# TensorE filler matmuls in the token routing, and MLP row groups written out in place of a loop

## What is computed

```python
scores = scale * q @ k.T            # 8 heads of 64; heads 0-3: last 32 keys, heads 4-7: every 4th of last 128
x = softmax(scores, mask) @ v       # -> (2304, 512)
expert_idx = argmax(logits); gate_w = softmax(logits)[expert_idx]     # logits: normalised x times 8 normalised rows / tau
y = gate_w * (relu(x @ w1[e]) @ w2[e])      # one of 8 experts per token, hidden width 1024
h = y @ w_in; out = (h * cos(h)) @ w_out    # hidden width 2048
```

## Time and profile before

| What | Value |
|---|---|
| Median of three runs | 880.99 us |
| The profiled execution, its own time | 879.44 us |
| Its span, first to last instruction | 877.5 us |
| Time outside the span (879.44 - 877.5) | 1.9 us |
| TensorE (PE) busy | 823.3 us, 94% |
| TensorE weight loads (PEld) busy | 745.4 us, 85% |
| VectorE (DVE) busy | 607.6 us, 69% |
| ScalarE (ACT) busy | 481.4 us, 55% |
| GpSimd (POOL) busy | 75.6 us, 9% |
| Mean granted TensorE clock | 0.978 |
| Share of TensorE in the chain that ended last | 78% |

### The profile page before, as it was taken

The page is one execution under the profiler, slowest core; times in us unless marked ns, Lnnn a source line. Parts: engine busy times, 40 slices in busy tenths (PEclk is TensorE's granted clock), DMA queues, the critical chain, the costliest instruction groups (busy, mean ns, idle before and its releaser), DMA issues.

```text
span 877.5 us, 15798 instructions
## 1 busy us (share of the span) xinstructions
PE 823.3 (94%) x4902; PEld 745.4 (85%) x4902; DVE 607.6 (69%) x1169; ACT 481.4 (55%) x919; POOL 75.6 (9%) x134
## 2 busy tenths in 40 slices
PE   5999999749999999999989999999999999999993
PEld 3787876439999999999988999988999988999992
DVE  6888886575555566455567777778777788777762
ACT  3557765315545545444456666676656676656651
POOL 4022112141001000000000000001000002000002
PEclk9999999959999999999999999999999999999998
DMA  6498986234444443444242122123212214121001
GB/s 138 93 221 181 193 198 184 70 109 156 129 165 163 144 129 119 139 144 144 73 145 73 49 73 71 51 63 130 72 49 71 72 48 145 48 72 59 14 0 72
DMA packets 114911, 93.67 MB, mean 107 GB/s; under 512 B 65816, under 2 KB 94488, under 8 KB 114848
## 3 DMA queue, kind: packets, MB, share of 16 engines
q1 hardware_dynamic: 109920, 78.81, 31.1%
q0 software_dynamic: 4928, 14.16, 4.9%
HBM read 83.51 MB, written 9.44 MB: 106 GB/s over the span
## 4 chain that ended last, share of the span: by engine, by line
PE 78%; DVE 7%; DMA 5%; issue 4%; ACT 3%; POOL 1%; DVEq 0%; ACTq 0%; POOLq 0%; SPq 0%
PE bank L687 23%; PE bank L689 23%; PE bank L688 23%; DMA xtok<-x_rows 3%; PE bank L585 2%; PE bank L564 2%; PE bank L638 2%; PE bank L729 1%; PE bank L573 1%; DMA x_rows<-osb 1%; PE bank L654 1%; PE bank L548 1%; ACT yh L1010 1%; DMA dn_raw<-in_moe_w_out_dram 1%; DVE row_max L1156 1%
## 5 line engine op out<-in xcount | busy, mean ns | idle before, releaser
L687 PE MATMUL bank<-yh,up_l 128*128 128x384 f32 x384 | 129.7, 338 | 2.4 <-DVE yl L1409 2.4
L689 PE MATMUL bank<-yh,up_h 128*128 128x384 f32 x384 | 130.1, 339 | 0.0
L688 PE MATMUL bank<-yl,up_h 128*128 128x384 f32 x384 | 129.4, 337 | 0.0
L687 PE MATMUL bank<-dn_h,hid 128*128 128x512 f32 x288 | 113.0, 392 | 4.5 <-DVE hid L1431 4.2
L689 PE MATMUL bank<-dn_h,hid 128*128 128x512 f32 x288 | 113.9, 395 | 0.0
L688 PE MATMUL bank<-dn_l,hid 128*128 128x512 f32 x288 | 113.7, 395 | 0.0
L1219 DVE TENSOR_TENSOR dn_l<-dn_raw,dn_h 128x512 fp32r<-128x512 f32 (+1 forms) x80 | 71.9, 900 | 53.3 <-ACT dn_h L905 53.3
L1025 ACT ACTIVATE work<-bank 128x384 f32<-128x384 f32 x96 | 47.2, 491 | 81.4 <-PE bank L689 78.4
L687 PE MATMUL bank<-xh,up_l 128*128 128x352 f32 x256 | 85.2, 333 | 1.7 <-DVE xl L1351 1.4
L1037 ACT ACTIVATE work<-work 128x384 f32<-128x384 f32 x96 | 50.4, 525 | 66.0 <-DVE work L1426 66.0
L1421 DVE TENSOR_SCALAR work<-work 128x384 f32<-128x384 f32 x96 | 34.5, 360 | 75.3 <-ACT work L1025 75.3
(11 more groups left out here) (194 smaller groups left out, 1659.1 us busy)
## 6 DMA issues: line engine op xcount, KB each, us to landing
up_raw<-in_moe_w_dram SPq DMA_DIRECT2D x32, 512.0 KB, 3.5
dn_raw<-in_moe_w_dram SPq DMA_DIRECT2D x32, 512.0 KB, 3.4
up_raw<-in_moe_w_in_dram SPq DMA_DIRECT2D x24, 512.0 KB, 3.2
dn_raw<-in_moe_w_out_dram SPq DMA_DIRECT2D x24, 512.0 KB, 3.4
qn<-in_q_dram SPq DMA_DIRECT2D x32, 144.0 KB, 2.8
kn<-in_k_dram SPq DMA_DIRECT2D x32, 144.0 KB, 3.3
xtok<-x_rows SPq DMA_DIRECT2D x4, 1152.0 KB, 7.5
x_rows<-osb POOLq DMA_DIRECT2D x8, 288.0 KB, 3.9
```

Of the source, the lines that this page charges most:

```text
L687: mm(o, w[1], x[0], start=first, stop=False, skip_group_check=True)
L688: mm(o, w[0], x[1], start=False, stop=False, skip_group_check=True)
L689: return mm(o, w[0], x[0], start=False, stop=last, skip_group_check=True)
```

## The change

Two edits. A helper `fill(n)` on TensorE issues n matmuls of the 128x128 float32 identity by itself into the first 128 columns of bank 4, which nobody reads. It is called at seven places of the routing, always between one step of TensorE and the next wait. And the three loops over m of the MLP become Python loops, so that the body stands in the program three times and each `If` on m is decided when the program is written.

```diff
         def before_this(eng, i, work):
 
+            if isinstance(i, int):
+                if i > 0:
+                    work()
+                return
             with eng.If(i > 0):
                 work()
...
             last.then_inc(logits_done, 1)
 
+            def fill(n):
+
+                for _ in range(n):
+                    mm(bank[4][:, 0:P], ident[:], ident[:], start=True, stop=True, skip_group_check=True)
+
+            fill(14)
             pe.wait_ge(onehot_ready, 1)
...
             mm(bank[5][:, RT * E:2 * RT * E], ones[:], oh, start=True, stop=True, skip_group_check=True).then_inc(counts_done, 1)
 
+            fill(48)
             for t in range(RT):
                 if t % LANE_TILES == 0:
                     pe.wait_ge(lanes_ready, t // LANE_TILES + 1)
...
             last.then_inc(row_ids_done, 1)
+            fill(28)
             pe.wait_ge(to_gate_ready, 1)
...
             last.then_inc(row_gates_done, 1)
+            fill(6)
...
             for tile in range(3):
                 transpose_rows(tile, tile)
+                fill((16, 2, 6)[tile])
             expert_block(0, 0)
...
-            with pe.Fori(0, NM) as m:
+            for m in range(NM):
                 for i in range(2 * FT2):
                     if i >= 2:
                         mlp_up(m, i)
                         mlp_dn(m, i - 2)
                     else:
-                        with pe.If(m > 0):
+                        if m > 0:
                             mlp_up(m, i)
                             mlp_dn(m, i - 2)
...
-            with act.Fori(0, NM) as m:
+            for m in range(NM):
...
-            with dve.Fori(0, NM) as m:
+            for m in range(NM):
```

More of the change, by code:

```diff
@@ L1008, in group_hi @@
             def group_hi(m, half):
-                m = m if isinstance(m, int) else within(m, NM - 1, "under m < NM - 1")
                 A(yh[half][:], X[:, :, bass.ds(m * MR + half * HR, HR)], ACT.Copy).then_inc(ml["in_hi"], 1)
@@ L1075, in _ @@
                     if i in (2 * FT2 - 3, 2 * FT2 - 1):
-                        with act.If(m < NM - 1):
+                        if m < NM - 1:
                             group_hi(m + 1, (i - 2 * FT2 + 3) // 2)
@@ L1088, in _ @@
                     if i == 0:
-                        with act.If(m < 1):
+                        if m < 1:
                             last_block_out()
@@ L1465, in _ @@
                     if i in (2 * FT2 - 3, 2 * FT2 - 1):
-                        with dve.If(m < NM - 1):
+                        if m < NM - 1:
                             group_lo(m + 1, (i - 2 * FT2 + 3) // 2)
@@ L1478, in _ @@
                     if i == 0:
-                        with dve.If(m < 1):
+                        if m < 1:
                             last_block_out()
```

## The result

| | Before | After |
|---|---|---|
| Median | 879.46 us (877.73 to 881.51, 8 runs) | 887.25 us (883.59 to 890.51, 8 runs) |
| The profiled execution, its span | 879.44, 877.5 us | 885.73, 883.9 us |
| Mean granted clock | 0.978 | 0.992 |

The ratio is 1.0085, 95% interval 1.0061 to 1.0108: slower. The direction was right and 887.25 lies in the range. The 2.25 us to the forecast of 885.0 hide larger misses of both signs: as a difference, 4.95 us were forecast, and the medians give 7.8.

A forecast was written before the change was run, and what follows sets the result against it. TensorE bounds the MLP; VectorE's chain and the gathering DMA bound the routing. Routing +5.55, clock +1.6 and loops -2.2 give +4.95 on 879.44, so 884.4, raised to 885.0 us partway toward the median 880.99; range 879.5 to 889.5.

The forecast's parts named there:

- The price of a fill: TensorE in the routing: each fill is two records of 0.109 us, 0.218 us in all.
- Both rivals of other prices: Routing fills: one record of 0.109 us or cheaper, about 877.5 us, chance 0.13; or 0.285 us, about 892, chance 0.09.
- The fills one by one, up to the gates: Routing on TensorE: fills overshoot their waits, making the counts 0.5 us late, the row numbers 2.5 and `gates` 5.4.
- `gates` stands at 192.3: Routing, after fill(28) and 24 matmuls: `gates` is ready at 192.3 instead of 186.85, late by 5.4 us.
- `fill(16)`, 3.49 us, at the full clock: Routing, between the transposes of tiles 0 and 1: the fill runs from 193.85 to 197.35.
- A new idle, and the clock: Before hidden tile 2: TensorE idles some 3.3 us, then a low-clock stretch of 3.4 us costs +1.6 us.
- the case without a fall: Rival for the new idle: no second fall of the clock, +3.35 us, about 883.3 us, chance 0.26.
- The loops, -2.2 us: MLP written out: two back edges give 2 x 1.0 us, register waits at the first group perhaps 0.2.
- Its rival, that nothing comes: MLP loops: 0 instead of -2.2 us, about 887 us, within the first case's range; no chance of its own.
- The whole low stretch is worth about 0.5 us: Routing: 27.3 us at the low clock cost only about 0.5 us on the path.
- The sum: Whole kernel: 5.55 + 1.6 - 2.2 = +4.95 us, from 879.44 to 884.4, stated as 885.0 us.

The follow-up runs named there:

- half_fills: The changed kernel with every count of fills halved (7, 24, 14, 3 and 8, 1, 3), MLP groups written out: 879.51 us, 1.0008 of before.
- repeat_after: The changed kernel once more, unchanged, for a second trace: 887.47 us, 1.0091 of the kernel before.
- fills_only: The changed kernel with its fills kept but the MLP's hardware loops restored: 892.33 us, 1.0145 of the kernel before.
- no_fill_behind_gates: The changed kernel without the fill(6) between row_gates_done and the first transposes: 888.59 us, 1.0111 of the kernel before.
- loops_only: The changed kernel without any fills, MLP groups written out: 876.34 us, 0.9970 of the kernel before.
- early_half: The changed kernel with only the first two fill calls, halved to fill(7) and fill(24), groups written out: 874.29 us, 0.9951 of the kernel before.
- wide_fills: The changed kernel with float32 fills of 512 columns, counts 2, 6, 4, 1 and 2, 0, 1: 876.67 us, 0.9975 of the kernel before.
- short_fills: The changed kernel with bf16 fills of 96x96 by 96 columns, counts 36, 128, 72, 16 and 40, 6, 16: 877.81 us, 0.9981 of before.
- transpose_fills: The changed kernel with full counts, each fill a float32 transpose of the identity, one record: 878.13 us, 0.9985 of the kernel before.

## Why the prediction was right, and where not

- **The price of a fill: right.** The trace holds 5142 - 4902 = 240 more records, two for each. 28 of them take 3.39 us, so (3.39 - 0.27) / 27 = 0.116 a record, and 96 give (10.91 - 0.27) / 95 = 0.112: 0.224 to 0.23 us a fill against my 0.218. Both rivals of other prices fall. By the 134 cycles a matmul of the Trainium skill, "TensorE: Matmul & The Clock Gate", section "Back-to-back issue gap", 0.056 us, 48 fills would take 2.7 us (an estimate), and 10.91 were measured. The same section calls that figure too low for a stream of weight loads and matmuls and gives about 81 ns there, which would be 3.9 us for the 48 (an estimate too).
- **The fills one by one, up to the gates: right.** Less the 1.0 us of the late start, the counts stood at 174.0 (forecast 173.8), VectorE took the row numbers at 185.8 (185.4), and the second 24 began at 191.9 (191.3). The gates matmuls ended at 192.7 (192.3).
- **"`gates` stands at 192.3": wrong, by 2.9 us.** 0.4 of it is TensorE; the rest is the late increment, 2.5 us where before had 0.11. The step took it that work on TensorE delays only what is queued behind it on TensorE. half_fills shows at its gates that this fails even where no fill overshoots.
- **`fill(16)`, 3.49 us, at the full clock: wrong, by 1.9 us.** The late increment leaves TensorE idle for 2.11 us, the clock falls 0.9 us after its end, and the fill takes 5.36 us. It stands ahead of the transposes of tile 1, whose rows were scaled by 197.8; VectorE waits 4.88 us for what follows, as the second fence above shows. From `gates` to hidden tile 2 it took 16.6 us (196.18 to 212.78), where before and in my forecast it was 14.8. 5.55 + 0.4 + 2.5 + 1.8 = 10.2, and 10.1 were measured.
- **"A new idle, and the clock", +1.6 us: wrong.** The idle came, 2.93 us against the 3.3 forecast (the 24 matmuls before it took 4.1 us and not 3.7), but the clock stayed at 1.00. It stayed so in repeat_after too and fell there in fills_only and no_fill_behind_gates (6.8 us each), all behind an idle of 2.93 or 2.94 us: two of four traces, where I had read one row as a rule. I had given the case without a fall 0.26. What happened was neither case: the fall came at another place.
- **The loops, -2.2 us: right, a little low.** loops_only gives -2.7 with an interval of -4.0 to -1.4 (0.3% of 879 and its bounds). Its rival, that nothing comes, falls. The branch's own time is no guide, as far as this case goes: by the about 51 and 108 ns of the Trainium skill, "Advanced Engine Details and Errata", section "Control Flow Timing", two back edges give 0.3 us (an estimate), and the two stalls of ScalarE of 1.45 us each went down to 0.2 each. The changed kernel gained another 1.6 us or so in the MLP, which is the missing low stretch at its start; I had not counted with it.
- **"The whole low stretch is worth about 0.5 us": small, as forecast; its size is not resolved.** It runs for 23.9 us in loops_only, 13.6 in early_half and 3.4 in wide_fills, and their routing takes 31.25, 31.0 and 31.2 us. Between before and loops_only, with the same code there, lie 0.85.
- **The sum** came near by luck: the routing cost 4.6 us more than forecast, the low stretch of 1.6 us did not come, the MLP and the experts gave some 2.6 us more (4.2 + 0.6 - 2.2), and 1.0 us came from the attention: 4.95 + 4.6 - 1.6 - 2.6 + 1.0 is the 6.4 between the spans. The stated 885.0 stood on a median of 880.99 for before, which eight runs put at 879.46.

## What to carry to other kernels

A raised clock is worth what TensorE's work on the critical path saves by it. Where TensorE served a chain on other engines, cutting the stretch at half the clock from 24 us to 3.4 changed the routing by less than two traces of the same code differ, and each filler matmul that overshoots its wait is paid in full, more so if it meets the low clock and takes twice as long. Compare with no fillers at all first: loops_only, 0.9970, was as good as the best kernel with fills all through the routing, wide_fills, 0.9975 (short_fills: 0.9981). If fillers are used, take a few wide matmuls that end before the wait even at the low clock, and look in the trace at the time from the end of a real matmul to the start of who waits for it, not only at TensorE's idles. A stall at a loop's back edge, on whichever engine shows "issue", can be removed by writing a short hardware loop out: 2.7 us for two back edges here.

## What the runs showed of the hardware that was not expected

- The increments of the gates matmuls (bf16) came 0.9 to 2.8 us after their recorded end and those of tile 1's transposes (float32) 1.2 to 2.7 us, behind float32 fill records of 0.11 us while the gathering DMAs ran; at the same two places without such fills it was some 0.1 us. Why stays open.
- The fall of the clock is not told by the idle alone. It fell after idles of 2.11 us (after, at 198.06) and 2.36 us (before, at 453.02), and stayed at 1.00 after 2.93 us (after, at 212.8) and after 2.33 us (early_half and after, at the MLP's start); in repeat_after, the same kernel as after with the same idle of 2.33 us there, it fell, at 463.87. In transpose_fills it fell at 184.5 without any long idle: from 181.3 on TensorE had done groups of six small matmuls, 0.32 us of every 0.87. These low stretches were 3.4 or 6.8 us long.
- This is part of the spread between runs of one kernel: the fastest run of the changed kernel, 883.59 us, had a mean clock of 0.994, the slowest, 890.51, had 0.989. By 3.4 us at half the clock, 0.0019 of the mean, that is 2.6 stretches more, at 1.7 us each at most 4.4 of the 6.9 us, an estimate.
- A plain float32 matmul is two records for 128 columns, of 0.112 to 0.116 us with weights of 128 columns, (10.91 - 0.27) / 95 and (3.39 - 0.27) / 27, and of 0.110 with weights of 32, (5.43 - 0.27) / 47.
